# Rows of x and the experts' inner values turned by 32x32 transposes of VectorE

## The chip, the cores and the metric

The program runs on one core of a Trainium2 chip. The metric is the device time of one execution in microseconds, the median of three runs. Five engines work side by side and meet through semaphores: TensorE (PE) multiplies matrices, VectorE (DVE) and ScalarE (ACT) do elementwise work, GpSimd (POOL) splits weights and issues the indirect transfers, SyncE (SP) issues plain transfers.

## What is computed

An attention with pooled keys gives `x` (2304 tokens, 512 columns); each token goes through two of eight experts and then through a dense layer:

```python
logits = x @ w_gate
noisy_logits = logits + np.log1p(np.exp(x @ w_noise)) * noise
top2 = np.argpartition(-noisy_logits, 2, axis=1)[:, :2]      # and softmax weights of the two
for e in range(E):                                           # 8 experts, w1 512x1024, w2 1024x512
    for k in range(2):
        mask = top2[:, k] == e
        h = np.maximum(x[mask] @ w1[e], 0.0)
        out[mask] += top2_w[mask, k, None] * (h @ w2[e])
h = out @ w_in                                               # 512x2048
return np.maximum(0.01 * h, h) @ w_out
```

## The kernel before

The span has three stages. First attention and gating (to about 115 us) over 18 tiles of 128 tokens; their rows are sent to `x_sorted` in DRAM, grouped by expert, by indirect transfers of GpSimd, which go on until 143 us. Then 43 blocks (`BLOCKS`) of 128 sorted rows, one after the other, each with one expert: this is the block loop that the change touches (115 to 659 us). Then the dense layer over five groups of tokens, which the change leaves alone.

All products are made in three passes of reduced precision: `hi` is a value rounded to float32r, `lo` the rest, and `halves3` (L730 to L732) issues hi x hi, hi x lo and lo x hi. So each block needs its rows and its inner values turned (the contracted dimension on the partitions) and split into hi and lo:

- `turn_rows(b)`, L737: four TensorE transposes 128x128 of `xs` (rows of the block) into PSUM bank 6. `copy_rows` (ScalarE, L987) makes `xs_hi`, `split_rows` (VectorE, L1273) makes `xs_lo`.
- `up(b)`: 24 matmuls 128x512 into banks 0 and 1 (two halves of 512 of the 1024 inner values).
- `relu(b)`, L993 (ScalarE): two passes from PSUM to `h_sb`. `turn_h(b)`, L756: eight TensorE transposes into banks 2 and 3. `copy_h` (ScalarE, L999) makes `hT_hi`, `split_h` (VectorE, L1280) makes `hT_lo`.
- `down(b)`: 24 matmuls 128x512 into bank 4. `copy_y` (VectorE, L1289) takes them to `y_sb`, `store_rows` (issued by ScalarE, L1004) writes them to `y_blocks`.
- `load_rows(b)` (issued by ScalarE, L983) brings the 128 rows of a block from `x_sorted` in one transfer of 256 KB.

The order is written out by hand, each engine's program runs in its own order. TensorE runs `up(b)`, `turn_rows(b + 1)`, `down(b - 1)`, `turn_h(b)` in a loop over b; blocks 0 to 4 stand ahead of the loop. VectorE has bookkeeping between its splits in the first blocks: `list_y_rows`, `finish_y_rows` (L1356 to L1365, L1224 to L1227) and `place_late` (L1371 to L1376). GpSimd splits the weights of an expert into hi and lo as soon as the expert two before it is done (L547, L549, 16 chunks), and at the end gathers the rows of each token from `y_blocks` (L606); the last two blocks' part of the first two tiles is added on TensorE instead (`add_late`, L778; `add_mixed`, L788).

## Time and profile before

| | us |
|---|---|
| median of 3 runs (lowest, highest) | 1072.41 (1072.01, 1073.37) |
| the profiled execution's own time | 1069.9 |
| its span | 1068.2 |
| TensorE busy | 1033.9 |
| GpSimd busy | 398.7 |
| VectorE busy | 360.8 |
| ScalarE busy | 272.3 |

The span is the time from the first to the last recorded instruction of the profiled execution; what lies around it is 1.7 us there. Busy time of a matmul runs past the start of the next one, since matmuls are pipelined; how far two follow each other is read from their starts or from the chain of waits. The chain is followed back from the last instruction: at each step to what released it, or to the instruction before it on its engine.

### The profile page before, as it was taken

Reading aid. Unit: us, or ns where it says so; the run is one execution under the profiler, and the core shown is the slowest. Engines: PE = TensorE matmul, PEld = TensorE weight load, DVE = VectorE, ACT = ScalarE, POOL = GpSimd, SP = SyncE. Lnnn points to the kernel's source line nnn. Section 1 sums busy time; section 2 is a strip of 40 time slices with the busy share of each in tenths; the row PEclk is TensorE's granted clock in tenths of the full one; section 3 lists DMA queues with packets and bytes.
Section 4 is the critical chain, followed back from the end, with each engine's and each line's share of the span. In section 5 each row is a group of like instructions: output and inputs, shape, how many; then the busy total and the mean of one; then the engine's idle time right before and its main releaser. Section 6 shows DMA issues by size and latency. Waiting matters only on the chain.

```text
span 1068.2 us, 16369 instructions
## 1 busy us (share of the span) xinstructions
PE 1033.9 (97%) x5222; PEld 871.3 (82%) x5223; DVE 360.8 (34%) x652; ACT 272.3 (25%) x498; POOL 398.7 (37%) x453
## 2 busy tenths in 40 slices
PE   5998889999999999999999999999999999999998
PEld 4988668888888888888888887888888888888886
DVE  5886624222222222221212224643323333333222
ACT  3542122222222222222222221322222222222222
POOL 6588880643719073462908208811101000000000
PEclk9997999999999999999999999999999999999999
DMA  8955561342515143351514315411101101001001
GB/s 307 341 179 195 190 202 43 118 119 87 157 49 176 59 137 109 94 151 56 171 59 147 98 39 168 119 41 40 37 4 62 38 20 60 21 1 40 1 1 40
DMA packets 53927, 106.06 MB, mean 99 GB/s; under 512 B 7424, under 2 KB 7552, under 8 KB 53888
## 3 DMA queue, kind: packets, MB, share of 16 engines
q1 hardware_dynamic: 35456, 63.59, 19.2%
q10 hardware_dynamic: 12672, 23.07, 6.7%
q0 software_dynamic: 5760, 18.88, 5.4%
q8 instruction: 24, 0.39, 0.2%
q14 instruction: 15, 0.12, 0.0%
HBM read 77.47 MB, written 28.05 MB: 99 GB/s over the span
## 4 chain that ended last, share of the span: by engine, by line
PE 88%; POOL 5%; DVE 2%; issue 2%; DMA 1%; ACT 0%; SPq 0%; ACTq 0%; POOLq 0%; DVEq 0%
PE ps L730 26%; PE ps L732 26%; PE ps L731 26%; PE ps L756 3%; POOL x_sorted L516 3%; PE ps L737 2%; PE ps L659 2%; PE ps L683 1%; POOL w_split L549 1%; PE ps L844 1%; POOL w_split L547 1%; PE ps L669 1%; DMA k_raw<-in_kT_dram 0%; POOL w_split L493 0%; DVE maxima L1108 0%
## 5 line engine op out<-in xcount | busy, mean ns | idle before, releaser
L549 POOL TENSOR_TENSOR w_split<-w_raw,w_split 128x512 fp32r<-128x512 f32 x144 | 186.2, 1293 | 12.0
L547 POOL TENSOR_SCALAR w_split<-w_raw 128x512 fp32r<-128x512 f32 x144 | 91.4, 635 | 217.4 <-PE ps L732 216.9
L730 PE MATMUL ps<-w_split,hT_hi 128*128 (+1 forms) x344 | 139.2, 405 | 1.2 <-DVE hT_lo L1280 1.2
L730 PE MATMUL ps<-w_split,xs_hi 128*128 (+1 forms) x344 | 137.6, 400 | 2.3 <-issue 2.3
L732 PE MATMUL ps<-w_split,hT_lo 128*128 (+1 forms) x344 | 135.1, 393 | 0.0
L731 PE MATMUL ps<-w_split,hT_hi 128*128 (+1 forms) x344 | 134.5, 391 | 0.0
L732 PE MATMUL ps<-w_split,xs_lo 128*128 (+1 forms) x344 | 134.2, 390 | 0.0
L731 PE MATMUL ps<-w_split,xs_hi 128*128 (+1 forms) x344 | 134.1, 390 | 0.0
L606 POOL DMA_INDIRECT y_in<-y_blocks,y_rows x36 | 34.9, 969 | 254.1 <-DVE x L1411 201.1
L730 PE MATMUL ps<-x_hi,w_split 128*128 128x512 f32 (+1 forms) x320 | 119.4, 373 | 0.6 <-DVE x_lo L1444 0.6
L732 PE MATMUL ps<-x_hi,w_split 128*128 128x512 f32 (+1 forms) x320 | 117.8, 368 | 0.0
L731 PE MATMUL ps<-x_lo,w_split 128*128 128x512 f32 (+1 forms) x320 | 117.8, 368 | 0.0
L1456 DVE TENSOR_TENSOR g_sb<-h_small,ps 128x512 f32<-128x512 f32 (+1 forms) x80 | 50.7, 634 | 192.7 <-ACT h_small L1078 192.5
L999 ACT ACTIVATE hT_hi<-ps 128x512 fp32r<-128x512 f32 x86 | 46.9, 597 | 264.9 <-PE ps L756 256.6
L730 PE MATMUL ps<-w_split,g_hi 128*128 128x512 f32 x288 | 112.5, 390 | 0.7 <-DVE g_lo L1459 0.7
L731 PE MATMUL ps<-w_split,g_hi 128*128 128x512 f32 x288 | 112.2, 390 | 0.0
L732 PE MATMUL ps<-w_split,g_lo 128*128 128x512 f32 x288 | 112.1, 389 | 0.0
L1078 ACT ACTIVATE h_small<-ps 128x512 f32<-128x512 f32 (+1 forms) x80 | 44.4, 555 | 221.8 <-PE ps L732 221.7
L1273 DVE TENSOR_TENSOR xs_lo<-ps,xs_hi 128x512 fp32r<-128x512 f32 x44 | 30.4, 691 | 172.2 <-ACT xs_hi L987 171.9
L993 ACT ACTIVATE h_sb<-ps 128x512 f32<-128x512 f32 x86 | 51.4, 599 | 144.2 <-PE ps L732 139.3
L1289 DVE COPY y_sb<-ps 128x512 f32<-128x512 f32 x42 | 29.0, 691 | 172.4 <-PE ps L732 172.4
L730 PEld LDWEIGHTS ps<-w_split,xs_hi 128*128 128x128 f32 x344 | 64.7, 188 | 14.8 <-issue 2.8
(176 smaller groups left out, 1514.5 us busy)
## 6 DMA issues: line engine op xcount, KB each, us to landing
w_raw<-in_wall_dram SPq DMA_DIRECT2D x160, 256.0 KB
xs<-x_sorted ACTq DMA_DIRECT2D x45, 256.0 KB
y_blocks<-y_sb ACTq DMA_DIRECT2D x43, 256.0 KB, 2.0
k_raw<-in_kT_dram SPq DMA_DIRECT2D x16, 288.0 KB, 5.1
q_sb<-in_qT_dram SPq DMA_DIRECT2D x18, 256.0 KB, 4.5
v_raw<-in_vT_dram SPq DMA_DIRECT2D x16, 288.0 KB, 5.9
out_dram<-h_sb SPq DMA_DIRECT2D x10, 256.0 KB, 2.0
x_sorted<-zero_rows SPq DMA_DIRECT2D x9, 256.0 KB, 4.2
```

The source lines that it names most:

```text
L516: pool.indirect_dma_start(out=x_sorted[:, :], out_offset=bass.IndirectOffsetOnAxis(ap=slots_i[:, tile, k:k + 1], axis=0), in_=x_rows[:, ti ...
L547: pool.tensor_scalar(hi, w_raw[:, a, :], 1.0, 0.0, ALU.mult, ALU.add).then_inc(split_hi, 1)
L549: pool.tensor_tensor(lo, w_raw[:, a, :], hi.bitcast(F32), ALU.subtract).then_inc(split, 1)
L606: pool.indirect_dma_start(out=y_in[:, t % YRING, k, :], out_offset=None, in_=y_blocks[0:rows, :], in_offset=bass.IndirectOffsetOnAxis(ap=y ...
L730: pe.matmul(out_ap, lhs_hi, rhs_hi, start=first, stop=False)
L731: pe.matmul(out_ap, lhs_hi, rhs_lo, start=False, stop=False)
L732: return pe.matmul(out_ap, lhs_lo, rhs_hi, start=False, stop=last)
L756: mm = pe.transpose(ps[:, HT_BANK + n, k * P:(k + 1) * P], h_sb[:, (4 * n + k) * P:(4 * n + k + 1) * P], ident[:, :])
L993: act.activation(h_sb[:, n * BANK:(n + 1) * BANK], ps[:, H_BANK + n, :], ACT.Relu).then_inc(h_relued, 1)
L999: act.activation(hT_hi[:, 4 * n:4 * n + 4, :].rearrange("p a b -> p (a b)"), ps[:, HT_BANK + n, :], ACT.Copy).then_inc(hT_hi_made, 1)
L1078: act.activation(h_small[:, f % 2, 0:n], ps[:, H2_BANK + f % 2, 0:n], ACT.Copy, scale=0.01).then_inc(h2_small, 1)
L1456: dve.tensor_tensor(g_sb[:, f % 2, 0:n], h_small[:, f % 2, 0:n], ps[:, H2_BANK + f % 2, 0:n], ALU.max).then_inc(g_made, 1)
```

## The change

TensorE's transposes of x (L737) and, but for block 0, of h (L756) are gone. A transpose on VectorE turns squares of 32x32 in place, so the rest of the turn is made by where the squares are read and written:

- x: a block's rows are loaded by four transfers (`load_by_quads`, 64 KB each, pieces of 512 bytes), one for each quarter of the columns, each to 32 partitions. One VectorE transpose of 128x512 from `xs` into bank 6 then gives x turned, with the contracted dimension in another order. The rows of w1 (and of w2, for h) are laid out in that order on the host.
- h: 16 VectorE transposes of 32 partitions x 256 elements each read banks 0 and 1 and write banks 2 and 3 (`turn_squares`; t is the quarter of the partitions that is read, a the one that is written). Eight stand in `turn_front`, behind the first half of `up`, eight in `turn_back`, behind the second, with `split_rows` of the next block after its first two. The relu is made behind the turn, in `relu_half` (ScalarE) and `split_half` (VectorE, maximum with 0 and subtraction in one).
- `copy_y` moves from VectorE to ScalarE.
- TensorE runs `up(b)`, `down(b - 1)`. Each half of `up(b)` now waits until the same bank of block b - 1 has been turned. The last `down` writes bank 6, and `add_late(0)` and `add_mixed(0)` stand in its middle.

```diff
--- before.py
+++ after.py
@@ -731,30 +735,26 @@
...
+            def up(b, expert, first=False):
...
                 for n in range(F // BANK):
+                    if not first:
+                        pe.wait_ge(h_turned, b * 2 + (n - 1))
...
-            def turn_h(b):
+            def turn_first_h():
+                pe.wait_ge(h_relued, 2)
                 for n in range(2):
-                    pe.wait_ge(h_relued, b * 2 + n + 1)
                     for k in range(4):
@@ -792,47 +792,40 @@
...
-                if not first:
+                if not first and not last:
                     pe.wait_ge(y_copied, b)
                 for k in range(KF):
-                    if first and k == KF // 2:
-                        turn_rows(b + 1)
+                    if last and k == KF // 2:
+                        pe.wait_ge(y_copied, BLOCKS - 1)
+                        pe.wait_ge(late_copied, 1)
+                        add_late(0)
+                        add_mixed(0)
                     if last and k == KF - 2:
                         add_mixed(1)
                     if k % 4 == 0:
                         pe.wait_ge(hT_split, b * 2 + k // 4 + 1)
...
+                    mm = halves3(ps[:, LAST_Y_BANK if last else Y_BANK, :], hT_hi[:, k, :], hT_lo[:, k, :],
...
+                    if k == KF // 2 - 1:
+                        mm.then_inc(half_down, 1)
...
-            turn_rows(0)
-            up(0, 0)
-            turn_h(0)
+            up(0, 0, True)
+            turn_first_h()
             down(0, 0, True)
             pe.wait_ge(lists_ready, 1)
             up(1, expert_of(1))
-            turn_rows(2)
-            turn_h(1)
             for b in range(2, LISTED_BY):
                 up(b, expert_of(b))
-                turn_rows(b + 1)
                 down(b - 1, expert_of(b - 1), False)
-                if b == LISTED_BY - 1:
-                    turn_late()
-                turn_h(b)
+            turn_late()
             with pe.Fori(LISTED_BY, BLOCKS) as b:
                 up(b, expert_of(b))
-                turn_rows(b + 1)
                 down(b - 1, expert_of(b - 1), False)
-                turn_h(b)
-            pe.wait_ge(y_copied, FIRST_LATE + 1)
-            pe.wait_ge(late_copied, 1)
-            add_late(0)
-            add_mixed(0)
             down(BLOCKS - 1, EXPERTS - 1, False, True)
             add_late(1)
@@ -978,26 +971,52 @@
...
+            def load_by_quads(row):
+
+                for a in range(QUADS):
+                    act.dma_start(xs[a * QUAD:(a + 1) * QUAD, :].rearrange("i (t c) -> i t c", t=QUADS),
+                                  x_sorted[bass.ds(row, P), a * P:(a + 1) * P].rearrange("(t i) c -> i t c", t=QUADS)
+                                  ).then_inc(xs_in, 16)
+
             def load_rows(b):
                 row = act.value_load(block_row[0:1, bass.ds(b, 1)], min_val=0, max_val=DUMMY)
-                act.dma_start(xs[:, :], x_sorted[bass.ds(row, P), :]).then_inc(xs_in, 16)
+                act.wait_ge(xs_turned, b)
+                load_by_quads(row)
...
+            def relu_half(n):
+                act.activation(hT_hi[:, 4 * n:4 * n + 4, :].rearrange("p a b -> p (a b)"),
+                               ps[:, HT_BANK + n, :], ACT.Relu).then_inc(hT_hi_made, 1)
+
+            def relu_front(b):
+                act.wait_ge(h_turned, b * 2 + 2)
+                act.wait_ge(half_down, b)
+                relu_half(0)
+
+            def relu_back(b):
+                act.wait_ge(blocks_done, b)
+                relu_half(1)
+
+            def copy_y(b, first=False):
+                act.wait_ge(blocks_done, b + 1)
+                if not first:
+                    act.wait_ge(y_out, b * 16)
+                act.activation(y_sb[:, :], ps[:, Y_BANK, :], ACT.Copy).then_inc(y_copied, 1)
+
+            def rows_used(b):
+                act.wait_ge(h_summed, b * 2 + 2)
 
...
             copy_rows(2)
+            relu_front(1)
+            store_rows(0)
+            relu_back(1)
             act.wait_ge(early_landed, 2)
             load_rows(3)
...
-            with act.Fori(LISTED_BY, BLOCKS) as b:
-                relu(b)
+            with act.Fori(LISTED_BY, BLOCKS - 1) as b:
+                copy_y(b - 2)
+                relu_back(b - 1)
+                store_rows(b - 2)
+                load_rows(b + 2)
+                rows_used(b)
                 copy_rows(b + 1)
-                load_rows(b + 2)
-                store_rows(b - 1)
-                copy_h(b)
+                relu_front(b)
+            copy_y(BLOCKS - 3)
+            relu_back(BLOCKS - 2)
+            store_rows(BLOCKS - 3)
+            relu_front(BLOCKS - 1)
+            copy_y(BLOCKS - 2)
+            relu_back(BLOCKS - 1)
+            store_rows(BLOCKS - 2)
@@ -1274,20 +1313,42 @@
...
+            def turn_rows(b, first=False):
+                dve.wait_ge(xs_in, b * (16 * QUADS) + 16 * QUADS)
                 if not first:
-                    dve.wait_ge(y_out, b * 16)
-                dve.tensor_copy(y_sb[:, :], ps[:, Y_BANK, :]).then_inc(y_copied, 1)
-
+                    dve.wait_ge(xs_split, b)
+                dve.transpose(ps[:, XT_BANK, :].rearrange("p (k t i) -> p t k i", k=KD, t=QUADS),
+                              xs[:, :].rearrange("p (t k i) -> p t k i", t=QUADS, k=KD)).then_inc(xs_turned, 1)
+
+            def turn_squares(squares):
+                for a, t in squares:
+                    ins = dve.transpose(
+                        ps[a * QUAD:(a + 1) * QUAD, HT_BANK:HT_BANK + 2, :]
+                        .rearrange("p n (k t i) -> p (n k) t i", t=QUADS, i=QUAD)[:, :, t, :],
+                        ps[t * QUAD:(t + 1) * QUAD, H_BANK + a // 2, a % 2 * (F // QUADS):(a % 2 + 1) * (F // QUADS)]
+                        .rearrange("p (k i) -> p k i", i=QUAD))
+                return ins
+
+            def turn_front(b):
+                dve.wait_ge(hT_split, b * 2)
+                dve.wait_ge(h_summed, b * 2 + 1)
+                turn_squares([(a, t) for a in (0, 1) for t in range(QUADS)]).then_inc(h_turned, 1)
+
+            def turn_back(b, rows):
+                dve.wait_ge(h_summed, b * 2 + 2)
+                turn_squares([(2, 0), (2, 1)])
+                if rows:
+                    split_rows(b + 1)
+                turn_squares([(2, 2), (2, 3), (3, 0), (3, 1), (3, 2), (3, 3)]).then_inc(h_turned, 1)
+
+            def split_half(b, n):
+                dve.wait_ge(hT_hi_made, b * 2 + n + 1)
+                dve.scalar_tensor_tensor(out=hT_lo[:, 4 * n:4 * n + 4, :].rearrange("p a b -> p (a b)"),
+                                         in0=ps[:, HT_BANK + n, :], scalar=0.0,
+                                         in1=hT_hi[:, 4 * n:4 * n + 4, :].rearrange("p a b -> p (a b)").bitcast(F32),
+                                         op0=ALU.max, op1=ALU.subtract).then_inc(hT_split, 1)
+
+            turn_rows(0, True)
@@ -1380,24 +1441,37 @@
...
+            turn_rows(2)
+            turn_front(1)
+            turn_back(1, True)
+            split_half(1, 0)
+            split_half(1, 1)
+            turn_front(2)
+            turn_back(2, False)
+            split_half(2, 0)
+            turn_rows(3)
             split_rows(3)
...
-            with dve.Fori(4, BLOCKS - 1) as b:
-                split_rows(b + 1)
-                copy_y(b - 1, False)
-                split_h(b)
...
+            with dve.Fori(LISTED_BY, BLOCKS - 1) as b:
+                turn_rows(b + 1)
+                split_half(b - 1, 1)
+                turn_front(b)
+                turn_back(b, True)
+                split_half(b, 0)
...
-            split_rows(BLOCKS)
+            split_half(BLOCKS - 2, 1)
+            turn_front(BLOCKS - 1)
+            turn_back(BLOCKS - 1, False)
+            split_half(BLOCKS - 1, 0)
             mix_tile(0)
-            copy_y(BLOCKS - 2, False)
-            split_h(BLOCKS - 1)
+            split_half(BLOCKS - 1, 1)
...
-    w1 = inputs['moe_w1'].reshape(EXPERTS, KD, P, F).transpose(0, 2, 1, 3).reshape(EXPERTS, P, KD * F)
-    w2 = inputs['moe_w2'].reshape(EXPERTS, KF, P, D).transpose(0, 2, 1, 3).reshape(EXPERTS, P, KF * D)
+    w1 = inputs['moe_w1'].reshape(EXPERTS, QUADS, KD, QUAD, F).transpose(0, 1, 3, 2, 4).reshape(EXPERTS, P, KD * F)
+    w2 = inputs['moe_w2'].reshape(EXPERTS, QUADS, KF, QUAD, D).transpose(0, 1, 3, 2, 4).reshape(EXPERTS, P, KF * D)
```

VectorE's program in the block loop. Before, one round (`xs_lo` is written by `split_rows`, `y_sb` by `copy_y`, `hT_lo` by `split_h`):

```order
L1273 TENSOR_TENSOR xs_lo<-ps,xs_hi 128x512
L1288 ISA
L1289 COPY y_sb<-ps 128x512
L1279 ISA
L1280 TENSOR_TENSOR hT_lo<-ps,hT_hi 128x512
L1279 REGISTER_ALU
L1280 TENSOR_TENSOR hT_lo<-ps,hT_hi 128x512
```

Now, the same engine and loop:

```order
L1320 STREAM_TRANSPOSE ps<-xs 128x4x4x32
L1345 ISA
L1346 SCALAR_TENSOR_TENSOR hT_lo<-ps,hT_hi 128x512
L1333 REGISTER_ALU
L1334 REGISTER_ALU
L1325 STREAM_TRANSPOSE ps<-ps 32x8x32 x8
L1338 REGISTER_ALU
L1325 STREAM_TRANSPOSE ps<-ps 32x8x32 x2
L1311 REGISTER_ALU
L1312 TENSOR_TENSOR xs_lo<-ps,xs_hi 128x512
L1325 STREAM_TRANSPOSE ps<-ps 32x8x32 x6
L1346 SCALAR_TENSOR_TENSOR hT_lo<-ps,hT_hi 128x512
```

The copy of y has left, 17 transposes have come, and the two splits of h now stand on either side of the turn of the next x.

TensorE's program in the block loop, between `up(b)` and `down(b - 1)`. Before (the rows of L810 read the block's expert, a register for the address of the weights):

```order
L731 MATMUL ps<-w_split,xs_hi 128x512
L732 MATMUL ps<-w_split,xs_lo 128x512
L735 ISA
L737 MATMUL ps<-ident,xs 128x128 x4
L810 ISA
L810 TENSOR_LOAD block_expert
L810 ISA x2
```

Now:

```order
L735 MATMUL ps<-w_split,xs_hi 128x512
L736 MATMUL ps<-w_split,xs_lo 128x512
L815 ISA
L815 TENSOR_LOAD block_expert
L815 ISA x2
L806 ISA
L734 ISA
L734 MATMUL ps<-w_split,hT_hi 128x512
```

The four transposes between the two groups of matmuls are gone, and the read of the expert stands directly behind the last matmul.

VectorE's program ahead of the loop, around block 4's `place_late` (it writes `code`, `x` and `h_small`). Before:

```order
L1289 COPY y_sb<-ps 128x512
L1280 TENSOR_TENSOR hT_lo<-ps,hT_hi 128x512 x2
L1371 TENSOR_SCALAR code<-slots_f 128x4
L1374 TENSOR_SCALAR x<-late_rows,code,mix 128x256 x2
L1376 TENSOR_TENSOR h_small<-x 128x256
L1374 TENSOR_SCALAR x<-late_rows,code,mix 128x256 x2
L1376 TENSOR_TENSOR h_small<-x 128x256
```

Now:

```order
L1346 SCALAR_TENSOR_TENSOR hT_lo<-ps,hT_hi 128x512
L1432 TENSOR_SCALAR code<-slots_f 128x4
L1435 TENSOR_SCALAR x<-late_rows,code,mix 128x256 x2
L1437 TENSOR_TENSOR h_small<-x 128x256
L1435 TENSOR_SCALAR x<-late_rows,code,mix 128x256 x2
L1437 TENSOR_TENSOR h_small<-x 128x256
L1325 STREAM_TRANSPOSE ps<-ps 32x8x32 x10
L1312 TENSOR_TENSOR xs_lo<-ps,xs_hi 128x512
L1325 STREAM_TRANSPOSE ps<-ps 32x8x32 x6
```

The bookkeeping now stands ahead of the block's 16 squares and of the split of block 5's rows, in place of standing behind all splits.

## Rows read from the trace of the kernel before

**Rows 1.** The page: busy time of TensorE, its granted clock, the chain by engine.
```profile
PE 1033.9 (97%) x5222; PEld 871.3 (82%) x5223; DVE 360.8 (34%) x652; ACT 272.3 (25%) x498; POOL 398.7 (37%) x453
PEclk9997999999999999999999999999999999999999
PE 88%; POOL 5%; DVE 2%; issue 2%; DMA 1%; ACT 0%; SPq 0%; ACTq 0%; POOLq 0%; DVEq 0%
```

**Rows 2.** The chain of waits, one round: start us, us, what.
```profile
299.01 0.44 PE ps L737 x4
...
304.94 0.87 PE ps L756 x8
...
311.28 0.44 PE ps L737 x4
...
317.21 0.87 PE ps L756 x8
```

**Rows 3.** ScalarE's timeline, that round: start, us, engine, line, idle before <-releaser.
```profile
300.24 0.34 ACTq L983 DMA_DIRECT2D xs<-x_sorted  x1
...
306.37 1.09 ACT L999 ACTIVATE hT_hi<-ps 128x512 fp32r<-128x512 f32 x2 [6.23 <-PE ps L756]
```

**Rows 4.** VectorE's timeline of that round.
```profile
300.17 0.69 DVE L1273 TENSOR_TENSOR xs_lo<-ps,xs_hi 128x512 fp32r<-128x512 f32 x1 [4.15 <-ACT xs_hi L987]
305.08 0.69 DVE L1289 COPY y_sb<-ps 128x512 f32<-128x512 f32 x1 [4.22 <-PE ps L732]
307.00 1.29 DVE L1280 TENSOR_TENSOR hT_lo<-ps,hT_hi 128x512 fp32r<-128x512 f32 x2 [1.23 <-ACT hT_hi L999]
```

**Rows 5.** VectorE's timeline elsewhere: independent copies, dependent pairs, a scalar_tensor_tensor.
```profile
120.52 0.52 DVE L1317 SCALAR_TENSOR_TENSOR probsT<-bnum,ps 1x360 f32<-1x360 f32 x1
...
149.47 0.45 DVE L1344 TENSOR_TENSOR probs<-slots_f,ps 128x288 f32<-128x288 f32 x1
149.96 0.45 DVE L1345 TENSOR_TENSOR probs<-probs,ps 128x288 f32<-128x288 f32 x1
...
658.63 0.42 DVE L1423 COPY y_sb<-ps 128x256 f32<-128x256 f32 x1 [4.80 <-PE ps L732]
658.97 0.41 DVE L1424 COPY y_sb<-ps 128x256 f32<-128x256 f32 x1
```

**Rows 6.** The start: ScalarE's timeline (block 2's load), then the chain of waits.
```profile
132.68 0.34 ACTq L1011 DMA_DIRECT2D xs<-x_sorted  x1
...
146.17 3.13 DMA xs<-x_sorted
149.34 0.94 PE ps L737 x4
...
157.25 0.87 PE ps L756 x8
...
182.24 0.87 PE ps L756 x8
```

**Rows 7.** VectorE's timeline: first and last of `finish_y_rows`, then of `place_late`.
```profile
160.25 0.46 DVE L1356 TENSOR_TENSOR ps<-ps,code 128x288 f32<-128x288 f32 x1
...
163.16 0.18 DVE L1227 TENSOR_TENSOR mix<-z_exp,gap_exp 128x18 f32<-128x18 f32 x1
...
172.53 0.16 DVE L1371 TENSOR_SCALAR code<-slots_f 128x4 f32<-128x4 f32 x1
...
174.98 0.42 DVE L1376 TENSOR_TENSOR h_small<-x 128x256 f32<-128x256 f32 x1
```

**Rows 8.** The end: timelines of ScalarE (store of block 40), GpSimd, VectorE.
```profile
637.16 0.36 ACTq L1004 DMA_DIRECT2D y_blocks<-y_sb  x1
...
662.33 1.01 POOL L606 DMA_INDIRECT y_in<-y_blocks,y_rows  x1 [0.81 <-issue]
...
667.24 0.50 DVE L1407 TENSOR_SCALAR y_in<-y_in,mix 128x512 f32<-128x512 f32 x1 [0.27 <-DMA y_in<-y_blocks,y_rows]
```

**Rows 9.** GpSimd's timeline: the first chunk of an expert's weights.
```profile
317.50 0.62 POOL L547 TENSOR_SCALAR w_split<-w_raw 128x512 fp32r<-128x512 f32 x1 [29.91 <-PE ps L732]
```

97 lines of the change are left out of this document (46 added, 51 removed).

## The prediction

> **What bounds the kernel now.** Read the page first: TensorE is busy 97% of the span at full granted clock nearly throughout, VectorE 34%, ScalarE 25%, and 88% of the chain that ended last is TensorE [rows 1]. So the end moves only with TensorE's own work, as long as nobody makes it wait. Then read the chain of waits over one round of the block loop [rows 2]. A round is 12.27 us (304.94 to 317.21) and has no wait in it: 24 matmuls of `down` (299.45 to 304.94, 5.49), eight transposes of h (0.87), 24 matmuls of `up` (305.81 to 311.28, 5.47), four transposes of x (0.44). Matmuls are 10.96, transposes 1.31. Rows of a whole matmul alone follow each other at 0.227, which is 10.90 for 48; the rest is the slower first matmuls behind each turn. VectorE has four operations in such a round, 0.69 each, and waits for most of it [rows 4].
>
> **TensorE's part.** The 12 transposes go from every round. It falls by 12.27 - 10.90 = 1.37 us, if `up` and `down` can now follow each other directly. Block 0 keeps its eight. All 1.31 us were on the path, since the chain shows them.
>
> **VectorE's part, in one round.** Added: 16 turns of 32 partitions x 256 elements and one turn of 128x512; taken away: the copy of y, which goes to ScalarE. No row shows a transpose on VectorE, so each needs bounds.
> - The nearest rows are the two copies 128x256 out of PSUM [rows 5]: 0.42 long, started 0.34 apart, because one starts before the other is done. Two dependent operations of 288 elements start 0.49 apart at 0.45 each [rows 5]: their length plus 0.04. So one square costs 0.34 if squares overlap, 0.42 + 0.04 = 0.46 if each waits for the one ahead. Both ends assume one element a cycle. I take 0.46: each square reads another quarter of the partitions than the one ahead, which no pair of overlapping rows does.
> - The upper end is a turn that takes two cycles per four-byte element: as long as 512 elements, 0.69 [rows 4], so 0.60 to 0.73 from start to start. The lower end is 0.27 (0.69 - 0.42, no fixed cost).
> - The turn of x: as any 128x512 from or to PSUM, 0.69 to 0.71.
> - `split_half` is now a scalar_tensor_tensor. That form takes 0.52 at 360 elements, a tensor_tensor 0.45 at 288 [rows 5], which is one element a cycle for both: nothing over the old 0.69.
>
> In the order of its engine VectorE's round is then: 16 squares (16s), `split_rows` between the tenth and the eleventh (0.69 + 0.04), the wait for ScalarE's relu of the first half (0.04 + 0.60 + 0.04), `split_half` 0.69, turn of x 0.61, second `split_half` 0.60: **16s + 3.31**. ScalarE's copy of y and second relu (0.50 apart [rows 3]) end beside the turn of x. With s = 0.46 that is 10.67, with 0.34 it is 8.75, against TensorE's 10.90. VectorE fits, by 0.23 us at s = 0.46. The point from which it decides is s = 0.474.
>
> The Trainium skill speaks to this choice (VectorE: DVE Perf Modes, Two Vector instructions with no wait between them): an instruction whose input or output starts in another group of 32 partitions than the last one's is held until all earlier ones have finished. No row of this trace has such a pair. By this rule all 15 steps between squares are held; without it the round is 8.75 and the sum below 8 us lower. The same page (The three transpose paths) has 311 ns for a 128x128 turn of VectorE, and its table of rules sends a 128x128 turn to TensorE. An estimate from it, with 128 more elements at the slope of the rows, is 0.44 a square, or 0.48 with the gap of 0.04, which would put VectorE 0.1 us a round over TensorE and the result near 1035.
>
> What hides the rest of the round: `up` of block b+1 needs `split_rows` (10s + 0.8 after the squares begin) and its second half the last square; `down` of b needs the two splits only 5 us later. ScalarE has five passes of 0.60 and five issues of 0.34 [rows 3], 4.7 us of 10.9. A load of x in four pieces is issued by 1.4 us instead of 0.34; it stands behind the store of y on its queue and is issued about 7 us before its turn, against 3.13 from issue to use now [rows 6]: hidden, unless the quarters take over twice as long. The copy of y moves from VectorE to ScalarE and no longer delays `down`, which waits for it only a round later. The weights' split on GpSimd waits 29.9 us for TensorE per expert now [rows 9]; an expert's five rounds get 6.9 us shorter, so 23 us are left.
>
> **The start (blocks 0 to 5), stepped through with s = 0.46.** Here VectorE also has its lists to make, and every step is serial. Blocks 0 and 1 start within 1.2 us of before: x turned by VectorE, ScalarE's copy and the split stand in a row, but the old wait of block 1 for x inside `down` is gone. Block 2's load is issued at 132.68 [rows 6], plus 1.05 for the last quarter, plus 3.13: 136.9; turn 0.71; then ten squares 4.6 and a split 0.69: `up(2)` at 142.9. Six squares, relu, two splits (5.0) put the squares of block 2 at 147.9; 16 of them 7.4, relu and split 1.4, turn, copy and split of block 3 2.1: `up(3)` at 158.8, where it is 158.12 now [rows 6] (now `down(1)` waits behind the turn of block 3's x until 149.34; then it no longer does, so that time is won back). Block 4's x is issued at 158.2, lands at 162.4; turn, split, then `finish_y_rows` 3.1 [rows 7], squares: `up(4)` at 172.1. Block 4 has `place_late` (2.9) [rows 7] ahead of its squares: `up(5)` at 185.6 against 183.11 [rows 6]. **Loss 2.5 us.** With s = 0.34 the same steps give 178.7, a gain of 4.4.
>
> **The loop**: from `up(5)` to `up(42)` 37 rounds, 37 x 12.27 = 454.0 now and 37 x 10.90 = 403.3 then: **gain 50.7**.
>
> **The end.** `up(42)`, `down(41)`, `down(42)` with the late products: one turn of h (0.87) less; the half split of block 42 can come some tenths late: gain 0.7. Then the tail on GpSimd: it is free 24.3 us after the store of block 40 (637.16 to 661.5) and only then gathers tile 2, for which VectorE already waits 0.27 us [rows 8]. The stretch from that store to the end of the blocks gets shorter by the turns (some 2 to 3 us), GpSimd's does not: **loss 2.3**.
>
> Sum: 2.5 - 50.7 - 0.7 + 2.3 = -46.6. The profiled execution's span of 1068.2 becomes 1021.6; its own time was 1069.9 and the median of the runs is 1072.41, 4.2 over the span, so I forecast 1025.8, **1026**.
>
> **Rivals.**
> 1. *VectorE becomes the bound, still faster.* s between 0.474 and 0.54, or small costs between its instructions (registers, waits) that no row of an idle engine shows. Each 0.01 of s is 0.16 a round over 37 rounds, with the start 6.6 us in all: 1046 at 0.50, 1059 at 0.52. For it: the margin is 0.23 of 10.9 us. Against: the value taken is already the serial one.
> 2. *Slower: the turn takes two cycles for four bytes.* At s = 0.54 the kernel is as fast as before; from there VectorE's longer round sets the time. With 0.60 it is 1112, with 0.73 the round is 15.0 and the time 1199. For it: no row bounds the rate of a turn. Against: every other 4-byte operation here goes at one element a cycle (0.27 us for 256 more). The page Vector Engine (DVE) Microarchitecture Reference of the Trainium skill, section The reshape front-end and per-opcode configuration, has the array keep one element per cycle per lane.
> 3. *Squares overlap (s = 0.34).* TensorE still sets the loop, the start gains: 1018.5.
> 4. *The change doesn't do what it says at the start: quarters land late.* If a load takes 6.3 instead of 3.13, blocks 3 and 4 wait: +8, 1034. From about 9 us the loop waits too.
> 5. *TensorE's rounds don't shrink to 10.90* because the read of the block's expert was hidden by transposes: with 0.1 us twice a round +7.6, 1034.
>
> **How the numbers follow.** Forecast with small misses (1021 to 1031) 0.38; rival 3 0.17; rival 4 or 5 0.09; rival 1 0.22; rival 2 0.14. The range takes forecast and rivals 3 to 5, and rival 1 to s = 0.51: 1015 to 1053. What is left out is rival 2 and the upper end of rival 1. A measurement of this kernel can tell about 0.2% (2 us) from no change. Faster 0.84, same 0.02 (s just at 0.54), slower 0.14.
>
> **What the profile of the changed kernel would show.** The turn of squares' mean and the distance of two starts: 0.42 to 0.45 and 0.46; at 0.34 rival 3, at 0.6 and more rival 2. In the chain of waits of the loop only matmuls, a round of 10.9; if VectorE's transposes stand in it and TensorE idles before `up` for `xs_lo`, rival 1 or 2. Idle time of TensorE of about 3 us each before `up` of blocks 3, 4 and 5, most of all on `xs_lo`. Loads of x long landed when the turn of x starts, except blocks 1 to 4. TensorE waiting for x2 of tile 2 for about 2 us right behind the blocks. The forecast is wrong above all if a square takes more than 0.47 from start to start.

## The result, and the profile after

The changed kernel takes **1045.12 us** (median of 4 runs, 1042.48 to 1048.28), the kernel before 1072.8 (1072.01 to 1073.37): ratio 0.9744, 95% interval 0.9715 to 0.9772. A second measurement of the same two gave 0.9754 (0.9716 to 0.9793). It is faster by 2.6%; the forecast was 1026, so two fifths of the expected gain of 46.6 us are missing. The time lies inside the stated range, but not for the reason that the forecast gives. The profiled run took 1042.48, its span is 1040.8 against 1021.6 in the working.

The page of the changed kernel, busy times, clock, the chain's two lines and three groups; what answers it is [rows 1]:

```profile
PE 996.2 (96%) x4710; PEld 824.3 (79%) x4711; DVE 675.8 (65%) x1324; ACT 246.9 (24%) x455; POOL 398.7 (38%) x453
...
PEclk9988689999999999999999999999999999999999
...
PE 46%; DVE 38%; issue 8%; ACT 3%; DMA 2%; DVEq 1%; ACTq 1%; SPq 0%; POOL 0%; POOLq 0%
DVE ps L1325 27%; PE ps L734 13%; PE ps L735 13%; PE ps L736 13%; DVE hT_lo L1346 3%; DVE xs_lo L1312 3%; PE ps L687 3%; ACT hT_hi L1000 2%; PE ps L663 2%; DVE ps L1320 2%; PE ps L673 1%; DMA xs<-x_sorted 1%; PE ps L837 1%; PE ps L728 1%; DVEq L1469 0%
...
L1325 DVE STREAM_TRANSPOSE ps<-ps 32x256 f32<-32x256 f32 x672 | 313.1, 466 | 15.1 <-PE ps L736 0.2
...
xs<-x_sorted ACTq DMA_DIRECT2D x176, 64.0 KB, 2.2
```

TensorE still counts as busy 96% of the span, but VectorE, 2% of the chain before, is now 38% of it, and 27% alone are the squares (L1325). The squares' mean is 466 ns, where the working had 0.42 us.

VectorE's timeline over one round of the block loop (start us, length us, engine, line, idle time before and its releaser); it answers [rows 4]:

```profile
308.90 4.75 DVE L1325 STREAM_TRANSPOSE ps<-ps 32x256 f32<-32x256 f32 x10
313.67 0.69 DVE L1312 TENSOR_TENSOR xs_lo<-ps,xs_hi 128x512 fp32r<-128x512 f32 x1
314.39 2.90 DVE L1325 STREAM_TRANSPOSE ps<-ps 32x256 f32<-32x256 f32 x6
317.96 0.69 DVE L1346 SCALAR_TENSOR_TENSOR hT_lo<-ps,hT_hi 128x512 fp32r<-128x512 f32 x1 [0.67 <-ACT hT_hi L1000]
318.68 0.73 DVE L1320 STREAM_TRANSPOSE ps<-xs 128x512 f32<-128x512 f32 x1
319.32 0.67 DVE L1346 SCALAR_TENSOR_TENSOR hT_lo<-ps,hT_hi 128x512 fp32r<-128x512 f32 x1
320.11 4.76 DVE L1325 STREAM_TRANSPOSE ps<-ps 32x256 f32<-32x256 f32 x10
```

A round is 11.21 us (308.90 to 320.11), and VectorE has one wait in it, the 0.67 for ScalarE's relu of the first half. Ten squares take 4.77 from the first start to the next operation's: **0.477 a square**, just over the 0.474 from which VectorE decides by the working. TensorE's row of idle time hardly shows it, because its gap is short. Its timeline where `down` ends and `up` begins (two whole matmuls elsewhere follow each other at 0.23):

```profile
594.52 0.39 PE L735 MATMUL ps<-w_split,hT_hi 128*128 x1
594.75 0.39 PE L736 MATMUL ps<-w_split,hT_lo 128*128 x1
595.18 0.49 PE L734 MATMUL ps<-w_split,xs_hi 128*128 x1
595.51 0.39 PE L735 MATMUL ps<-w_split,xs_hi 128*128 x1
595.74 0.40 PE L736 MATMUL ps<-w_split,xs_lo 128*128 x1
```

Around the first matmul of `up` the starts stand 0.43 and 0.33 apart instead of 0.23: 0.3 us a round, 37 times, under "busy 96%". The busy share could not have told.

The start. VectorE's timeline at the split of blocks 0, 1 and 5 and at the turns for blocks 1 and 2; then ScalarE's issues of the loads of blocks 1 and 2 (four quarters each), which answer [rows 6]; then TensorE at `up` of block 0 and behind it:

```profile
118.64 0.69 DVE L1312 TENSOR_TENSOR xs_lo<-ps,xs_hi 128x512 fp32r<-128x512 f32 x1 [0.66 <-ACT xs_hi L988]
...
135.56 0.73 DVE L1320 STREAM_TRANSPOSE ps<-xs 128x512 f32<-128x512 f32 x1 [4.58 <-DMA xs<-x_sorted]
136.95 0.69 DVE L1312 TENSOR_TENSOR xs_lo<-ps,xs_hi 128x512 fp32r<-128x512 f32 x1 [0.66 <-ACT xs_hi L988]
...
141.95 0.73 DVE L1320 STREAM_TRANSPOSE ps<-xs 128x512 f32<-128x512 f32 x1 [2.36 <-DMA xs<-x_sorted]
...
190.15 0.69 DVE L1312 TENSOR_TENSOR xs_lo<-ps,xs_hi 128x512 fp32r<-128x512 f32 x1
```

```profile
130.79 1.89 ACTq L977 DMA_DIRECT2D xs<-x_sorted  x4
...
137.54 1.77 ACTq L977 DMA_DIRECT2D xs<-x_sorted  x4
```

```profile
119.39 0.80 PE L734 MATMUL ps<-w_split,xs_hi 128*128 128x512 f32 x1 [3.21 <-DVE xs_lo L1312]
128.37 1.09 PE L756 MATMUL ps<-ident,h_sb 128*128 128x128 f32 x8 [0.69 <-ACT h_sb L995]
```

From the start of `up` of block 0 to the transpositions behind its relu it is 9.0 us, where 24 matmuls take 5.5 in the loop: behind the idle 3.21 us the granted clock in 120 to 125 us is 0.51, the 1.2 GHz level.

### The profile page after: what moved, and what is told of

The parts are those of the page before. It is cut to its first block, busy times and chain, and to the rows that moved or that the text cites. A ratio compares the mean times of both kernels' runs of the same rounds, so it can differ in the third digit from the quotient of the medians.

```text
span 1040.8 us, 16475 instructions
## 1 busy us (share of the span) xinstructions
PE 996.2 (96%) x4710; PEld 824.3 (79%) x4711; DVE 675.8 (65%) x1324; ACT 246.9 (24%) x455; POOL 398.7 (38%) x453
## 4 chain that ended last, share of the span: by engine, by line
PE 46%; DVE 38%; issue 8%; ACT 3%; DMA 2%; DVEq 1%; ACTq 1%; SPq 0%; POOL 0%; POOLq 0%
DVE ps L1325 27%; PE ps L734 13%; PE ps L735 13%; PE ps L736 13%; DVE hT_lo L1346 3%; DVE xs_lo L1312 3%; PE ps L687 3%; ACT hT_hi L1000 2%; PE ps L663 2%; DVE ps L1320 2%; PE ps L673 1%; DMA xs<-x_sorted 1%; PE ps L837 1%; PE ps L728 1%; DVEq L1469 0%
## 5 line engine op out<-in xcount | busy, mean ns | idle before, releaser
L1325 DVE STREAM_TRANSPOSE ps<-ps 32x256 f32<-32x256 f32 x672 | 313.1, 466 | 15.1 <-PE ps L736 0.2
L734 PE MATMUL ps<-w_split,xs_hi 128*128 (+1 forms) x344 | 141.7, 412 | 15.2 <-DVE xs_lo L1312 13.9
L734 PE MATMUL ps<-w_split,hT_hi 128*128 (+1 forms) x344 | 134.9, 392 | 3.8 <-DVE hT_lo L1346 3.8
L736 PE MATMUL ps<-w_split,xs_lo 128*128 (+1 forms) x344 | 137.3, 399 | 0.0
L735 PE MATMUL ps<-w_split,xs_hi 128*128 (+1 forms) x344 | 137.2, 399 | 0.0
L735 PE MATMUL ps<-w_split,hT_hi 128*128 (+1 forms) x344 | 134.4, 391 | 0.0
L1000 ACT ACTIVATE hT_hi<-ps 128x512 fp32r<-128x512 f32 x86 | 51.6, 602 | 268.2 <-DVE ps L1325 267.4
L1535 DVE TENSOR_TENSOR g_lo<-g_sb,g_hi 128x512 fp32r<-128x512 f32 (+1 forms) x80 | 53.8, 672 | 52.5 <-ACT g_hi L1122 52.5
L734 PEld LDWEIGHTS ps<-w_split,hT_hi 128*128 128x128 f32 x344 | 65.0, 189 | 17.8 <-DVE hT_lo L1346 4.4
```

What stands on the lines that cost most here:

```text
L734: pe.matmul(out_ap, lhs_hi, rhs_hi, start=first, stop=False)
L735: pe.matmul(out_ap, lhs_hi, rhs_lo, start=False, stop=False)
L736: return pe.matmul(out_ap, lhs_lo, rhs_hi, start=False, stop=last)
L1000: act.activation(hT_hi[:, 4 * n:4 * n + 4, :].rearrange("p a b -> p (a b)"), ps[:, HT_BANK + n, :], ACT.Relu).then_inc(hT_hi_made, 1)
L1325: ins = dve.transpose(ps[a * QUAD:(a + 1) * QUAD, HT_BANK:HT_BANK + 2, :] .rearrange("p n (k t i) -> p (n k) t i", t=QUADS, i=QUAD)[:, :, ...
L1535: dve.tensor_tensor(g_lo[:, f % 2, 0:n], g_sb[:, f % 2, 0:n], g_hi[:, f % 2, 0:n].bitcast(F32), ALU.subtract).then_inc(g_split, 1)
```

## The experiments

Since traces differ in when the first block begins, each run is read in four stretches, all from VectorE's timeline: the start of the first split of x; from there to the split of block 5; from there to the split of block 42 (37 rounds); from there to the end of the span. The steady round stands beside them. "To block 5" has the five blocks of the start in it, "to the end" the last block and the dense layer.

| kernel | first split | to block 5 | 37 rounds | to the end | steady round | median us |
|---|---|---|---|---|---|---|
| changed | 118.6 | 71.5 | 415.2 | 435.5 | 11.21 | 1045.1 |
| changed, again | 117.1 | 71.9 | 415.0 | 437.0 | 11.21 | 1043.9 |
| earlier turn of x | 113.9 | 73.6 | 402.2 | 434.8 | 10.86 | 1026.1 |
| the same, again | 118.8 | 70.8 | 402.2 | 434.8 | 10.86 | 1029.0 |
| + 8 instead of 14 matmuls while VectorE picks | 116.5 | 70.4 | 402.2 | 434.9 | 10.86 | 1025.7 |
| earlier turn + matmuls ahead of block 0 + other order in blocks 1 to 4 | 121.7 | 69.1 | 402.2 | 434.8 | 10.86 | 1029.3 |
| the same + 8 instead of 14 matmuls | 116.1 | 68.4 | 402.2 | 435.5 | 10.86 | 1026.0 |
| eight matmuls ahead of block 0 | 119.0 | 70.0 | 415.0 | 435.6 | 11.21 | 1041.6 |
| h alone by VectorE | 112.9 | 71.3 | 418.5 | 435.0 | 11.37 | 1041.0 |
| x alone by VectorE | 124.1 | 58.6 | 436.1 | 436.0 | 11.77 | 1051.9 |
| one load of x | 118.7 | 68.8 | 415.0 | 435.6 | 11.21 | 1039.8 (one run) |
| squares in one quarter | 118.4 | 67.0 | 399.8 | 434.8 | 10.88 | 1021.6 (one run) |
| half squares | 118.2 | 64.8 | 399.3 | 435.4 | 10.88 | 1019.4 (one run) |

**1. What sets the loop.** The turn of x is taken into VectorE's wait for the relu.

```diff
+            turn_rows(LISTED_BY + 1)
-            with dve.Fori(LISTED_BY, BLOCKS - 1) as b:
-                turn_rows(b + 1)
+            with dve.Fori(LISTED_BY, BLOCKS - 2) as b:
                 split_half(b - 1, 1)
                 turn_front(b)
                 turn_back(b, True)
+                turn_rows(b + 2)
                 split_half(b, 0)
...
```

> Edit: in the block loop VectorE turns x of the block after next between its last square and the first half split of h, where it now waits 0.67 us for ScalarE's relu; until now that turn stood behind the split. Nothing else changes: same instructions, same counts. Theory A (the loop is set by VectorE's own serial chain, 16 squares at 0.477, four operations of 0.7, and its wait of 0.67 for the relu): the wait is filled, VectorE's round falls from 11.21 to about 10.55, TensorE's 48 matmuls (10.90) set the loop, 37 rounds of 0.31 less: about 11.5 us faster than the changed kernel, 1031 to 1036. TensorE then has no wait for xs_lo left in the loop. Rival B (the 11.21 comes from TensorE, from slower matmuls or from reading registers, and VectorE only follows it): a round stays at 11.2 and the time within 2 us of the changed kernel. Rival C (the turn of x so early waits for its load, issued only 4 to 5 us before): the turn shows a wait for DMA and the round gets no shorter or longer, 1045 or more.

Measured 1026.1 (1025.88 to 1029.19), ratio to the kernel before 0.9572 (0.9544 to 0.96). VectorE's timeline of one round:

```profile
302.64 4.75 DVE L1325 STREAM_TRANSPOSE ps<-ps 32x256 f32<-32x256 f32 x10
307.41 0.69 DVE L1312 TENSOR_TENSOR xs_lo<-ps,xs_hi 128x512 fp32r<-128x512 f32 x1
308.13 2.91 DVE L1325 STREAM_TRANSPOSE ps<-ps 32x256 f32<-32x256 f32 x6
311.07 0.73 DVE L1320 STREAM_TRANSPOSE ps<-xs 128x512 f32<-128x512 f32 x1
311.83 0.69 DVE L1346 SCALAR_TENSOR_TENSOR hT_lo<-ps,hT_hi 128x512 fp32r<-128x512 f32 x1
312.68 0.69 DVE L1346 SCALAR_TENSOR_TENSOR hT_lo<-ps,hT_hi 128x512 fp32r<-128x512 f32 x1 [0.16 <-ACT hT_hi L1000]
313.50 4.75 DVE L1325 STREAM_TRANSPOSE ps<-ps 32x256 f32<-32x256 f32 x10
```

The wait of 0.67 is filled by work, the round is 10.86, and `up`'s first matmul follows `down`'s last at 0.23 again. Theory A's round holds, with the same squares at the same 0.477: what decided was the sum of VectorE's serial chain, and 37 rounds give 13.0 us, not 11.5. Rival B falls, and so does rival C, for no turn of x in the loop waits for its load. The time itself came out 5 us under the expected 1031 to 1036: block 0 began 4.8 us earlier than in the changed kernel's profile, though nothing was edited there (experiment 5). In the start, which the edit doesn't touch either, the turn for block 2 came 4.69 us late in this profile, waiting for its load (2.57 in the repetition, expected as follows).

> Edit: the earlier turn of x in the loop once more, beside the two kernels built on it, because what comes before the first block differs by some us from one execution to the next. Theory A: the round is 10.86 again; from the first split of x to the end of the span 908 to 911 us again; median 1026 to 1029. Rival B (its 910.6 was a lucky landing of block 2's rows): more than 2 us away from it.

Measured 1028.95 (1025.37 to 1031.05), 907.8 from the first split to the end of the span where the first profile had 910.6: 2.8 us away, so by its own condition rival B, and the round is 10.86 again. So the round is sure to 0.01, and the stretch before it is not better known than some 3 us from one profile.

**2. Why a square costs 0.477.** The same sizes, but each square stays in the quarter it reads (h is then not truly transposed).

```diff
-                        ps[a * QUAD:(a + 1) * QUAD, HT_BANK:HT_BANK + 2, :]
-                        .rearrange("p n (k t i) -> p (n k) t i", t=QUADS, i=QUAD)[:, :, t, :],
+                        ps[t * QUAD:(t + 1) * QUAD, HT_BANK:HT_BANK + 2, :]
+                        .rearrange("p n (k t i) -> p (n k) t i", t=QUADS, i=QUAD)[:, :, a, :],
...
-                turn_squares([(a, t) for a in (0, 1) for t in range(QUADS)]).then_inc(h_turned, 1)
+                turn_squares([(a, t) for t in range(QUADS) for a in (0, 1)]).then_inc(h_turned, 1)
...
-                turn_squares([(2, 0), (2, 1)])
+                turn_squares([(2, 0), (3, 0)])
...
-                turn_squares([(2, 2), (2, 3), (3, 0), (3, 1), (3, 2), (3, 3)]).then_inc(h_turned, 1)
+                turn_squares([(2, 1), (3, 1), (2, 2), (3, 2), (2, 3), (3, 3)]).then_inc(h_turned, 1)
```

> Edit: the same 16 squares with the same sizes and columns, but each is written to the quarter of the partitions that it reads, and they are taken in pairs that stay in one quarter: of the steps between squares half keep the quarter of input and output, the other half change it. h is then not really transposed, so what the experts give differs from the reference. Theory A (a square that starts in another quarter than the last one is held until that one has ended): steps within a pair take 0.34 to 0.38 from start to start, steps between pairs stay at 0.477; VectorE's round falls by about 8 x 0.13 = 1.0 us to 10.2 and TensorE sets the loop with 10.9; one run of about 1031. Rival B (a transposition is always serial, whatever the quarter): all steps stay at 0.477, the round stays 11.2, about 1045.

One run of 1021.62. VectorE's timeline of a round:

```profile
309.15 4.06 DVE L1325 STREAM_TRANSPOSE ps<-ps 32x256 f32<-32x256 f32 x10 [0.83 <-PE ps L736]
313.13 0.66 DVE L1312 TENSOR_TENSOR xs_lo<-ps,xs_hi 128x512 fp32r<-128x512 f32 x1
313.82 2.45 DVE L1325 STREAM_TRANSPOSE ps<-ps 32x256 f32<-32x256 f32 x6
```

Ten squares now take 3.98 to the next start instead of 4.77, six take 2.45 instead of 2.90. The first three of the ten by themselves (the first two are a pair in one quarter, the third changes it):

```profile
309.15 0.45 DVE L1325 STREAM_TRANSPOSE ps<-ps 32x256 f32<-32x256 f32 x1 [0.83 <-PE ps L736]
309.52 0.41 DVE L1325 STREAM_TRANSPOSE ps<-ps 32x256 f32<-32x256 f32 x1
309.94 0.46 DVE L1325 STREAM_TRANSPOSE ps<-ps 32x256 f32<-32x256 f32 x1
```

The second starts 0.37 after the first, 0.08 before that one has ended; the third starts 0.01 after the end of the second. All pairs of the round are like these: 0.37 to 0.39 within a pair, and a change of quarter always behind the end of the one ahead (0.42 to 0.47 from start to start). In the changed kernel, where each step changes the quarter, each square starts 0.01 to 0.03 after the end of the one ahead, 0.47 to 0.50 from start to start. Theory A holds as to what makes a square wait. That steps between pairs stay at 0.477 was wrong, and the time is 9 us under its 1031, of which 4.5 are in the start. And now VectorE waits 0.83 for TensorE, whose bare round is thereby seen: 10.88. The Trainium skill states this (VectorE: DVE Perf Modes, Two Vector instructions with no wait between them): an instruction starts only when all earlier ones have finished if its input or output begins in another group of 32 partitions. The trace agrees: 0.01 us behind the end where the quarter changes, 0.08 ahead of it where it doesn't. A true transposition moves 16 squares between 4 quarters and 4 others, so no order of them keeps both quarters from one to the next.

What a square is made of, with half of its elements left out:

```diff
-                        .rearrange("p n (k t i) -> p (n k) t i", t=QUADS, i=QUAD)[:, :, t, :],
+                        .rearrange("p n (k t i) -> p (n k) t i", t=QUADS, i=QUAD)[:, 0:KF // 2, t, :],
...
-                        .rearrange("p (k i) -> p k i", i=QUAD))
+                        .rearrange("p (k i) -> p k i", i=QUAD)[:, 0:KF // 2, :])
```

> Edit: each of the 16 squares turns only 128 of its 256 elements a partition; the other half of h keeps old values, so the experts' values differ from the reference. What one square's price is made of: by the slope between a copy of 256 and an operation of 512 elements (0.42 and 0.69, 0.27 for 256 more) a square takes 0.466 - 0.13 = 0.33 and starts 0.34 after the last one. Theory A (fixed cost of about 0.2 plus one element a cycle): 0.33. Rival B (a turn pays more than one cycle an element, and a smaller fixed cost): 0.25 to 0.30. Both put VectorE's round under 9.2, so TensorE sets the loop with 10.88 a round as in the run with squares in one quarter; rival C (TensorE's own round is longer when VectorE turns whole squares) would give another round than 10.88.

VectorE's rows by tile (min, median and max of one, in ns), then its timeline:

```profile
L1325 DVE STREAM_TRANSPOSE ps<-ps x54: 319/332/347, 300.1 to 334.5; 32x128 f32<-32x128 f32 x54
```
```profile
306.87 3.42 DVE L1325 STREAM_TRANSPOSE ps<-ps 32x128 f32<-32x128 f32 x10 [0.82 <-PE ps L736]
310.31 0.69 DVE L1312 TENSOR_TENSOR xs_lo<-ps,xs_hi 128x512 fp32r<-128x512 f32 x1
```

332 ns against 466: 134 for 128 elements, 1.05 ns each, and 0.20 us fixed. The slope is the one between the copy of 256 and the operation of 512 elements (0.42 and 0.69). That is theory A, and with 16 squares 3.2 us of fixed cost a round. TensorE's round is 10.88 again, so rival C falls.

**3. The two halves of the change.** First h alone: x is turned by TensorE, with one load, as before.

```diff
+            def turn_rows(b):
+                pe.wait_ge(xs_in, b * 16 + 16)
+                for k in range(KD):
+                    mm = pe.transpose(ps[:, XT_BANK, k * P:(k + 1) * P], xs[:, k * P:(k + 1) * P], ident[:, :])
+                mm.then_inc(xs_turned, 1)
...
                 up(b, expert_of(b))
+                turn_rows(b + 1)
...
```

> Edit: half of the change. x is turned by TensorE again, four transposes behind each `up`, with one load of 256 KB and w1 laid out as before the change; only h is turned by VectorE. Theory A (VectorE's round 11.21 binds, TensorE's is 10.90): VectorE's round falls by its turn of x (0.64) to 10.57, TensorE's rises by 0.44 to 11.34: a round of 11.34 to 11.4, 37 rounds cost 5 to 6 us against the changed kernel, and the start gets back what quartered loads and VectorE's turns took (about 2 us): 1046 to 1050. Rival B (the turn of x on VectorE is nearly free because it lies beside waits): the round is 11.4 and the start is unchanged, 1051 or more. Rival C (the squares alone are slower than 0.477 when TensorE transposes into PSUM beside them): a round over 11.5, 1056 or more.

Then x alone, on the kernel before:

```diff
-                act.dma_start(xs[:, :], x_sorted[bass.ds(row, P), :]).then_inc(xs_in, 16)
+                load_by_quads(row)
...
             def split_rows(b):
+                dve.wait_ge(xs_in, b * (16 * QUADS) + 16 * QUADS)
+                if not isinstance(b, int) or b:
+                    dve.wait_ge(xs_split, b)
+                dve.transpose(ps[:, XT_BANK, :].rearrange("p (k t i) -> p t k i", k=KD, t=QUADS),
+                              xs[:, :].rearrange("p (t k i) -> p t k i", t=QUADS, k=KD)).then_inc(xs_turned, 1)
```

> Edit, made on the kernel before: the other half of the change. x comes by quarters, is turned by VectorE ahead of each split, and w1 is laid out for it; h is still turned by TensorE and copied by ScalarE, y is still copied by VectorE. Theory A (where TensorE sets the round, each transposition taken from it gives its own time, and VectorE has room): a round of 12.27 - 0.44 = 11.83, 37 rounds give back 16.3 us; the quartered loads and VectorE's turn in a row with copy and split cost 2 to 4 us in blocks 1 to 4: 1058 to 1060. Together with h alone (11.31 a round) that would show that the two halves add on TensorE (12.27 - 0.44 - 0.96 = 10.87, which the kernel with the earlier turn reached) and do not add in the changed kernel, 11.21, because VectorE is full. Rival B (VectorE's turn of x, waited for by ScalarE's copy, makes `up` wait for xs_lo in each round): a round over 12.0 and 1065 or more.

h alone: 1041.0 (1038.6 to 1044.2), ratio 0.9709 (0.9676 to 0.9743). x alone: 1051.85 (1049.62 to 1056.49), ratio 0.9795 (0.9763 to 0.9827). The rounds, from VectorE's timelines: with h alone its squares start at 302.18, 313.55 and 324.93, each time behind a wait for TensorE; with x alone it rests most of the round:

```profile
302.18 4.75 DVE L1327 STREAM_TRANSPOSE ps<-ps 32x256 f32<-32x256 f32 x10 [0.64 <-PE ps L736]
...
313.55 4.75 DVE L1327 STREAM_TRANSPOSE ps<-ps 32x256 f32<-32x256 f32 x10 [0.64 <-PE ps L736]
```
```profile
300.94 0.69 DVE L1274 TENSOR_TENSOR xs_lo<-ps,xs_hi 128x512 fp32r<-128x512 f32 x1 [3.48 <-ACT xs_hi L983]
...
312.72 0.69 DVE L1274 TENSOR_TENSOR xs_lo<-ps,xs_hi 128x512 fp32r<-128x512 f32 x1 [3.48 <-ACT xs_hi L983]
```

TensorE's round of 12.27 falls by 0.90 with h and by 0.50 with x: 10.87 with both, if they add, and 10.86 to 10.88 is what the kernels reach in which VectorE has room. In the changed kernel they give 1.06 instead of 1.40, and the missing 0.35 is VectorE's. The turn of x gave 0.16 us a steady round there (3.4 over the 37, since the first rounds of h alone are shorter), and nothing up to block 5 (71.3 against 71.5 and 71.9). Both theories' loops were right to 0.1 us, both times were missed. h alone was expected at 1046 to 1050 and is not told apart from the changed kernel (the intervals overlap); in its profile block 0 begins 5.8 us earlier than in the changed kernel's. x alone came out 6 us under the expectation: its round was 0.06 shorter than worked out (2.2 us), and in place of a loss of 2 to 4 us in the start its profile has 58.6 to block 5 where the kernel before has 61.2.

**4. What the start lost.** Eight matmuls ahead of the first `up` keep TensorE at work in its wait.

```diff
+            for _ in range(8):
+                pe.matmul(ps[:, HT_BANK, :], w_split[:, 0:P], w_split[:, 0:BANK], start=True, stop=True)
             up(0, 0, True)
```

> Edit: eight matmuls whose result nobody reads, ahead of the first `up`, in the time in which TensorE waits for the first xs_lo. Theory A (part of the 5.6 us that the start took longer than forecast is TensorE's clock, which the trace shows at the 1.2 GHz level behind each idle stretch): up(0) follows at 0.227 a matmul instead of 0.43 for its first 4 us, about 2 to 3 us earlier at its end; if block 1 hangs on down(0) and not on VectorE the kernel gets 2 to 3 us faster, 1042. Rival B (block 1's squares and splits wait for VectorE's own list work, not for TensorE): up(0) is faster but up(1) starts at the same 138.1 and the time is the same within 1 us, 1045.

Measured 1041.59 (1039.05 to 1045.23). TensorE's timeline:

```profile
119.75 0.50 PE L734 MATMUL ps<-w_split,xs_hi 128*128 128x512 f32 x1 [1.29 <-DVE xs_lo L1314]
126.21 1.09 PE L756 MATMUL ps<-ident,h_sb 128*128 128x128 f32 x8 [0.69 <-ACT h_sb L997]
```

From the start of `up` of block 0 to the transpositions it is 6.5 instead of 9.0 us, with the granted clock at 1.00 in 119.7 to 125 us. Block 5 is reached in 70.0 instead of 71.5 to 71.9: 1.5 to 1.9 us of the 2.5 are kept. The rest is lost ahead of the load of block 1: it is issued at 129.35, 1.4 us behind block 0's relus instead of 0.6; what held it is not shown. Both theories are half right. In whole times it can't be told from noise.

With one load of 256 KB in place of the quarters (the columns of x then stand in another order than the rows of w1):

```diff
-                for a in range(QUADS):
-                    act.dma_start(xs[a * QUAD:(a + 1) * QUAD, :].rearrange("i (t c) -> i t c", t=QUADS),
-                                  x_sorted[bass.ds(row, P), a * P:(a + 1) * P].rearrange("(t i) c -> i t c", t=QUADS)
-                                  ).then_inc(xs_in, 16)
+                act.dma_start(xs[:, :], x_sorted[bass.ds(row, P), :]).then_inc(xs_in, 16)
```

> Edit: x comes by one load of 256 KB instead of four quarters, while VectorE's turn stays; the columns then stand in another order than w1 expects, so the experts' values differ from the reference. Theory A (quarters cost 1.5 us of issue and show only where VectorE waits for the load, blocks 1, 2 and 4): those waits of 4.58, 2.36 and 2.71 shrink by about 1.2 each, ScalarE's issue group is 0.34 instead of 1.8, the loop stays at 11.21 a round; 1 to 3 us in all between the first split of x and block 5's. Rival B (the four strided transfers also slow the landing): the waits shrink by 2 or more each, 4 to 6 us in all. Rival C (in the loop the loads do matter): the round falls under 11.1.

One run of 1039.8. ScalarE's issue of block 1's load, and VectorE's turn of it:

```profile
129.92 0.36 ACTq L976 DMA_DIRECT2D xs<-x_sorted  x1
```
```profile
133.09 0.73 DVE L1317 STREAM_TRANSPOSE ps<-xs 128x512 f32<-128x512 f32 x1 [2.98 <-DMA xs<-x_sorted]
```

From the beginning of the issue to the turn it is 3.17 us, with quarters 4.77 (130.79 to 135.56): 1.5 of these 1.6 are issue (1.89 against 0.36), the landing is not slower. Block 1's wait shrinks by 1.60, block 4's by 0.77, block 2's not at all. Block 5 is reached in 68.8, 2.7 to 3.2 us sooner, of which 0.9 had come before the issue: TensorE's clock rose earlier in `up` of block 0 (0.70 against 0.50 in the first 5 us), which the edit doesn't touch. So the load is worth about 2 us. Theory A; the loop stays at 11.21, so rivals B and C fall.

Then the order of blocks 1 to 4: block 1's load ahead of block 0's relus, block 3's turn and split between block 2's squares. The run has the earlier turn and the eight matmuls ahead of block 0 as well.

```diff
+            for _ in range(8):
+                pe.matmul(ps[:, HT_BANK, :], w_split[:, 0:P], w_split[:, 0:BANK], start=True, stop=True)
             up(0, 0, True)
...
             relu_first()
+            act.wait_ge(lists_ready, 1)
+            act.wait_ge(first_known, 2)
+            load_early(1, early_landed)
...
             turn_front(2)
+            dve.wait_ge(h_summed, 6)
+            turn_squares([(2, 0), (2, 1)])
+            turn_rows(3)
+            turn_squares([(2, 2), (2, 3), (3, 0), (3, 1)])
+            split_rows(3)
+            turn_squares([(3, 2), (3, 3)]).then_inc(h_turned, 1)
+            split_half(2, 0)
+            split_half(2, 1)
+            finish_y_rows()
+            turn_rows(4)
...
```

> Edit: the earlier turn of x in the loop and the eight matmuls ahead of the first `up`, both as before, and the start in another order: the load of block 1 is issued ahead of block 0's relus, the turn and split of block 3's x stand between block 2's squares, the lists behind both splits and ahead of the next turn. Theory A (in blocks 1 to 5 TensorE waits for VectorE's serial order and for loads issued late, so another order gives it back): up(3) comes about 3.4 us earlier after up(2), up(5) 3 to 5 us earlier from the first split of x (67 to 70 instead of 73.6 with the earlier turn alone, 71.5 in the changed kernel), the loop stays at 10.86: 1021 to 1024. Rival B (the start hangs on GpSimd's scatter of the rows and on landing times, not on the order): up(5) stays at 71 to 74 from the first split and the time is 1026 as with the earlier turn alone.

Measured 1029.27 (1026.61 to 1033.95): by the whole time theory A missed. By the stretches: 69.1 from the first split to block 5, as expected, but the repetition of the earlier turn alone has 70.8 there, so 1.7 are gained and not 4.5. And the eight matmuls by themselves gave 1.5 to 1.9 in this stretch, so no gain of the new order is shown. By blocks it shifts time instead: the split of block 1 comes 2.9 us sooner behind that of block 0, that of block 2 then 3.6 later (block 0's second relus now stand behind the issue of the load, and VectorE waits 3.34 us for TensorE ahead of block 1's squares), that of block 3 2.2 sooner, where 3.4 were expected. And the first split came at 121.7, which no edit explains.

**5. What comes before the first block.** That stretch moved by 8 us between the profiles of kernels that are the same up to there (113.9 to 121.7); h alone (112.9) and x alone (124.1) lie outside, with an edit in the load and the turn of block 0's x.

> Edit: none, the changed kernel once more. The traces so far differ by up to 6 us before the first block: the first split of x comes at 118.6 in the changed kernel, at 113.9 with the earlier turn and at 112.9 with h alone, though nothing was edited there. Theory A (that stage varies from one execution to the next with TensorE's clock): the round is 11.21 again, the time between the first split of x and that of block 5 is 70 to 72.5, and the first split of x stands anywhere from 112 to 119, so that the median lands between 1040 and 1047. Rival B (each build has its own fixed place for it): 118.6 again and 1045 again.

Measured 1043.86 (1042.74 to 1050.54); first split at 117.1, 71.9 to block 5, round 11.21. Theory A as far as it goes. Part of it can be read: 16 matmuls of the last tiles, in the changed kernel and in its repetition:

```profile
101.24 3.68 PE L687 MATMUL ps<-v_pool,probsT 73*128 73x82 f32 x16 [1.48 <-DVE gate_prod L1172]
```
```profile
101.25 2.01 PE L687 MATMUL ps<-v_pool,probsT 73*128 73x82 f32 x16 [1.48 <-issue]
```

They start at the same time and take 3.68 us at a granted clock of 0.50 or 2.01 at 0.95, and the first split comes 1.6 us apart. The larger part lies earlier and stays open: these 16 start anywhere from 100.1 to 108.1. Later, while VectorE picks, TensorE runs 14 matmuls that only keep it busy (5.87 us at 109.51 in the changed kernel), and the last ranks start behind these at 115.22, when their picks had been ready since 112.81. So I left six of the 14 out:

```diff
-BUSY_AT = tuple((LINKS_BEFORE_LAST + n, 3) for n in (1, 4, 7, 10)) + ((LINKS_BEFORE_LAST + 13, 2),)
+BUSY_AT = tuple((LINKS_BEFORE_LAST + n, c) for n, c in ((1, 2), (4, 2), (7, 2), (10, 1), (13, 1)))
```

> Edit: the earlier turn of x in the loop, and of the 14 matmuls that keep TensorE busy while VectorE picks for the last three tiles only 8. At the 1.2 GHz level the 14 take 5.3 to 6.0 us and end 1.6 to 2.4 us after the picks are ready, so that the ranks of the last rows, and with them block 0, wait behind them. Theory A: the ranks start as soon as the picks are ready, the first split of x comes about 2 us earlier after the last picks, and the rest is as with the earlier turn alone: 1024. Rival B (with fewer matmuls TensorE's clock stays low for longer, and `up` of block 0 loses what the ranks gained): 1026 to 1028.

Measured 1025.65 (1024.49 to 1026.36), ratio 0.9559 (0.9528 to 0.9589). TensorE's timeline:

```profile
108.55 3.54 PE L728 MATMUL ps<-w_split 128*128 128x512 f32 x8 [1.34 <-DVE ps L1213]
...
112.94 0.40 PE L697 MATMUL ps<-picked,before 128*128 128x24 f32 x2 [0.84 <-DVE picks_sum L1241]
```

The ranks now wait for their picks and not for the eight. From the picks (112.89) to the first split it is 3.6 us, with 14 it was 5.2 in the kernel beside it (113.63 to 118.79) and 5.8 in the changed one. But these 1.6 us are not all gain, for the picks themselves came late in this profile:

```profile
111.46 1.21 DVE L1240 TENSOR_TENSOR picked<-picks 128x24 f32<-128x24 f32 x1
```

In the two kernels compared this step takes 0.18. From its start to the first split it is 5.0 us with eight matmuls and 4.9 in the last run below, 5.6 and 6.2 in the two compared and 5.2 to 7.1 in the ten profiles with 14 in which VectorE turns x. In two of these ten the step took 1.2 and 1.3 us as well, and there it is 5.2 and 5.3: beside them the eight matmuls gain 0.2 to 0.3. So the wait that was removed is shown, its worth is anything from 0.2 to 1.4 us, and the medians beside each other (1025.65 and 1028.95) go the same way with overlapping intervals.

> Edit: the run with the other order in blocks 1 to 4 (it took 906.1 from the first split of x to the end of the span, where the earlier turn alone took 910.6 and the changed kernel 922.2 and 923.9), and of the 14 matmuls only 8, as in the run beside it. Theory A (both gains stand, and what came before the first split in that run was chance): 906 from the first split to the end of the span, 2 us less before it: 1020 to 1023. Rival B (the other order gives back later what it gained, or the ranks' gain is lost by the clock): 1026 or more.

Measured 1026.01 (1023.9 to 1027.09), ratio 0.9567 (0.9536 to 0.9598). First split to the end 906.1 as expected, 116.1 before it; the whole is no better than with eight matmuls in place of 14 alone. Of the 2.0 us gained up to block 5 the end gives 0.6 back: the first half of the last `down` runs at a granted clock of 0.62 and takes 1.6 longer than with the earlier turn alone (1.00, behind the same 1.9 us of waiting), the rest of the end 0.9 less. The remainder is not told apart from noise. Rival B by the time. **The lowest median of this study is 1025.7**, 1.9% less than the changed kernel and 4.4% less than the kernel before. It isn't told apart from 1026.0 here and 1026.1 for the earlier turn alone: what is shown to matter is the place of one turn.

## Why the prediction was right and wrong

- **TensorE's part: right.** 10.90 a round was worked out, 10.86 to 10.88 is what it takes wherever VectorE has room, and both halves add. Rival 5 (a hidden read of the expert) is out. But that TensorE would set the loop of the changed kernel was wrong.
- **VectorE's round: the step that failed.** Worked out 16 x 0.46 + 3.31 = 10.67; the trace has 16 x 0.477 + 3.58 = 11.21. Of the miss of 0.54, 0.27 are the squares (0.466 long instead of 0.42, 0.01 between them) and 0.27 the fixed part, in which 0.79 instead of 0.60 pass from the last split to the next round's squares, across the loop's branch. Serial squares were forecast rightly; they were priced as a copy of the same size. Either error of 0.27 alone is more than the margin of 0.23. That is rival 1, with the square at its lower edge and the small costs between instructions that it names. With the true fixed part VectorE sets the round from (10.88 - 3.58) / 16 = 0.456 a square on, so the forecast's own 0.46 would have been over it. The estimate from the figure of the Trainium skill (VectorE: DVE Perf Modes, The three transpose paths; it is given for bf16), 0.44 long and 0.48 from start to start, lay nearer to 0.466 and 0.477 than my 0.42 and 0.46. The 1035 beside it doesn't follow from it: 0.1 us in 37 rounds and some 1 us in the start give 1031. Rival 1's 1046 and 1059 are 3 us too high by the same sum. The measured 1045 has the longer fixed part and the start in it.
- **The loop: 11.9 us of the 19.2 by which the span exceeds the working** (415.15 for 37 rounds instead of 403.3). That VectorE and not something else took them is shown by the first experiment.
- **The start: 5.6 us more** (`up(5)` at 191.24 instead of 185.6). 1.7 of it lie before block 0 and are within what this stretch varies by. The rest is nearly all between the splits of blocks 0 and 1, 18.3 us instead of about 14.4 (14.3 in the kernel before): 1.5 to 1.9 by the low clock behind TensorE's idle time (the experiment with eight matmuls), which the working did not count, and 1.6 by the load of block 1 in quarters, whose issue takes 1.9 us and starts only behind both relus, while VectorE waits 4.58 for it. Some 0.5 us stay open. That quarters cost only their issue was right; the issue was priced at 1.4 us and takes 1.8 to 1.9, and it was not hidden for blocks 1 and 4. Blocks 2 to 5 came about as stepped: 10.6, 16.3, 12.5, 13.8 against 10.8, 15.9, 13.3, 13.5.
- **The end: 1.5 us more.** TensorE waits 2.81 for block 42's last split, and its clock falls once more behind it (0.66 granted in 620.4 to 624.6):

```profile
620.38 0.80 PE L734 MATMUL ps<-w_split,hT_hi 128*128 128x512 f32 x1 [2.81 <-DVE hT_lo L1346]
620.97 0.63 PE L735 MATMUL ps<-w_split,hT_hi 128*128 128x512 f32 x1
```

  From `up(42)` on that is 3.6 more than worked out, and the loss of 2.3 us on GpSimd's gather [rows 8] came as 0.2: VectorE waited 0.24 for tile 2 at 640.17, for the stretch had not become shorter. The sum of the misses is 5.6 + 11.9 + 3.6 - 2.1 = 19.0, the 19.2 but for rounding.
- **Rivals 2, 3 and 4.** A turn does not cost twice what a copy costs an element (1.05 ns each). Squares don't overlap in this kernel, and the reason given was the true one, the change of quarter. Quarters don't land late, they are issued late.
- The chances: "faster" was right, and 1045 lies inside 1015 to 1053, by rival 1, whose part up to 0.51 the range had taken in. The likeliest case was not the one that came, and the sign that was named for it (more than 0.47 from start to start) did appear. With a margin of 2% of the round on an engine none of whose new rows existed, rival 1 deserved as much as the forecast.

## What to carry to other kernels

When work moves from a full engine to an idle one, add up the idle engine's whole serial chain, waits and loop branch included, and compare it with the new round of the other: where they come within a few per cent (here 2%), treat it as the bound, and look in the same step for an independent operation to put into its wait (here that gave 13 us in the loop, on top of the 28 of the change). A page that shows the first engine busy 96% doesn't contradict this; the share of the chain does, and the distance of starts at the seam between two stages. And where TensorE idles ahead of a stage, as here for 3 us, price the matmuls behind it at the low clock too.

## What the runs showed of the hardware

- A VectorE turn of 32 partitions x 256 fp32 from PSUM to PSUM takes 466 ns, of 128 elements 332 (0.20 fixed and 1.05 ns an element); one of 128 x 512 from SBUF to PSUM takes 727, where a subtraction of that size takes 692.
- When the quarter of the partitions changes, such a turn starts 0.01 to 0.03 us after the end of the one ahead (0.477 from start to start in the changed kernel); when it doesn't, it starts about 0.08 before that end (0.37 to 0.39 from start to start).
- Four loads of 64 KB are issued by ScalarE's queue in 1.8 to 1.9 us mostly (2.9 to 3.8 for block 3's), one of 256 KB in 0.34 to 0.36. The turn starts 2.9, 2.6 and 1.6 us behind the last issue with quarters (blocks 1, 2 and 4), 2.8, 4.1 and 2.2 with one load.
- One and the same group of 16 small matmuls took 2.01 us at a granted clock of 0.95 and 3.68 at 0.50 in two executions of one kernel, and the stretch before the first block varied by 8 us between kernels that are the same up to there. Medians of four runs don't tell 2 us apart in this kernel; the steady round repeats to 0.01 us.
